# Attention turn of a fused attention and two-layer kernel: pooled work moved ahead of local work, sums moved to the end on DVE, and epsilon held in a column that a reduction adds

## The reference

```python
# attention: two parts, added
q_d, k_d, v_d = means over groups of 4 positions           # 144 positions
out_d = softmax(scale * q_d @ k_d.T) @ v_d                 # pooled part
out_up = repeat(out_d, 4)
scores = where(|i - j| < 4, scale * q @ k.T, -1e9)         # local part: a band of 7 keys
out_local = softmax(scores) @ v
x = out_up + out_local                                     # 2304 tokens x 512
# softmax everywhere: e = exp(s - max); e / (sum(e) + 1e-9)
# first layer: h = x @ w_in (512 x 2048); g = h * tanh(softplus(h)); y = g @ w_out
# second layer: h = y @ w_in (512 x 1024); h * softmax(h); layer norm * g_ln; @ w_out
```

## Time and profile before

| what | value |
|---|---|
| median of 3 runs | 707.73 us (707.36 to 709.15) |
| profiled execution, its own time | 707.11 us |
| its span in the trace | 705.3 us |
| PE busy | 678.3 us (96%), 5098 matmuls |
| DVE busy | 369.9 us (52%), 675 instructions |
| ACT busy | 262.5 us (37%) |
| POOL busy | 183.2 us (26%) |

### The profile page before, as it was taken

The page is one execution under the profiler, slowest core; times in us unless marked ns, Lnnn a source line. Parts: engine busy times, 40 slices in busy tenths (PEclk is TensorE's granted clock), DMA queues, the critical chain, the costliest instruction groups (busy, mean ns, idle before and its releaser), DMA issues.

```text
span 705.3 us, 12609 instructions
## 1 busy us (share of the span) xinstructions
PE 678.3 (96%) x5098; PEld 626.7 (89%) x5098; DVE 369.9 (52%) x675; ACT 262.5 (37%) x583; POOL 183.2 (26%) x220
## 2 busy tenths in 40 slices
PE   5878799999999999999999999999999999999998
PEld 5667689999999999999999999999778888888886
DVE  8999966642223222322232332664796667756671
ACT  5788874321112111211121112136564444535441
POOL 5989820000000000000000000574535434354100
PEclk9999999999999999999999999999999999999999
DMA  7887783000000000000000030002000000000001
GB/s 239 234 236 221 209 309 147 1 1 0 1 1 1 1 0 1 1 1 1 0 2 1 1 119 1 1 1 90 31 16 16 30 31 16 16 31 30 31 16 45
DMA packets 25657, 37.51 MB, mean 53 GB/s; under 512 B 2944, under 2 KB 13184, under 8 KB 25472
## 3 DMA queue, kind: packets, MB, share of 16 engines
q1 hardware_dynamic: 25600, 36.72, 16.3%
HBM read 31.99 MB, written 4.72 MB: 52 GB/s over the span
## 4 chain that ended last, share of the span: by engine, by line
PE 82%; DVE 10%; issue 3%; ACT 2%; POOL 2%; DMA 1%; SPq 0%; DVEq 0%; ACTq 0%; POOLq 0%
PE psum L685 28%; PE psum L671 28%; PE psum L778 12%; PE psum L755 11%; PE psum L764 2%; DVE prob L1110 2%; DVE mx L1107 1%; DVE xy L1134 1%; ACT pprob L839 1%; DVE den L1124 1%; DVE psum L1098 1%; POOL ylo L548 1%; DMA qkT<-kT_dram 1%; DVE so L1296 1%; DVE kd L1073 1%
## 5 line engine op out<-in xcount | busy, mean ns | idle before, releaser
L1193 DVE CAST ghi<-g_sb 128x384 fp32r<-128x384 f32 x96 | 39.6, 413 | 245.5 <-PE psum L685 188.8
L894 ACT ACTIVATE g_sb<-psum 128x384 f32<-128x384 f32 x96 | 47.0, 490 | 292.6 <-PE psum L671 288.3
L671 PE MATMUL psum<-xhi,whi 128*128 128x384 f32 x384 | 129.7, 338 | 1.3 <-ACT g_sb L894 0.7
L671 PE MATMUL psum<-xlo,whi 128*128 128x384 f32 x384 | 129.1, 336 | 0.0
L685 PE MATMUL psum<-ghi,whi 128*128 128x384 f32 x384 | 129.1, 336 | 0.0
L685 PE MATMUL psum<-ghi,wlo 128*128 128x384 f32 x384 | 129.1, 336 | 0.0
L671 PE MATMUL psum<-xhi,wlo 128*128 128x384 f32 x384 | 129.1, 336 | 0.0
L685 PE MATMUL psum<-glo,whi 128*128 128x384 f32 x384 | 129.1, 336 | 0.0
L520 POOL TENSOR_TENSOR t<-raw 128x1024 f32<-128x1024 f32 x1 | 2.6, 2609 | 350.3 <-PE psum L685 350.3
L671 PEld LDWEIGHTS psum<-xhi,whi 128*128 128x128 f32 x384 | 72.3, 188 | 2.4 <-ACT g_sb L894 1.2
L685 PEld LDWEIGHTS psum<-glo,whi 128*128 128x128 f32 x384 | 72.3, 188 | 0.1
(11 more groups left out here) (123 smaller groups left out, 1052.2 us busy)
## 6 DMA issues: line engine op xcount, KB each, us to landing
wraw<-w_dram SPq DMA_DIRECT2D x12, 512.0 KB, 8.1
qkT<-qT_dram SPq DMA_DIRECT2D x16, 288.0 KB, 3.7
qkT<-kT_dram SPq DMA_DIRECT2D x16, 288.0 KB, 5.1
out_dram<-ob SPq DMA_DIRECT2D x18, 256.0 KB, 2.0
v<-v_dram SPq DMA_DIRECT2D x16, 256.0 KB
vw<-v_dram SPq DMA_DIRECT2D x32, 128.0 KB, 3.2
wraw<-w_dram SPq DMA_DIRECT2D x16, 256.0 KB, 6.3
raw<-w_dram SPq DMA_DIRECT2D x1, 2048.0 KB, 7.2
```

What stands on the lines that cost most here:

```text
L671: ins = nc.tensor.matmul(bank, a[:, w], b[:, kdx, :], start=(kdx == 0 and n == 0), stop=(kdx == KD - 1 and n == 2))
L894: nc.scalar.activation(g_sb[:, f % HR, :], psum[:, HB1 + f % HB, 0:N1], ACT.Mish).then_inc(g_ok, 1)
L1193: nc.vector.tensor_copy(ghi[:, f % GR, :], g_sb[:, f % HR, :]).then_inc(ghi_ok, 1)
```

## The change

On POOL `den` is filled with epsilon first. It gets a last axis of two: column 0 takes the sums, column 1 keeps epsilon for the whole kernel. The addition becomes a reduction over that axis into a new tensor `dsum`, and the reciprocal reads `dsum`. ACT and DVE wait once for the fill. On PE the pooled scores go ahead of the local ones. On ACT `exp_pooled` goes ahead of the eviction of the older unit and of `exp_local`; what stood after `exp_pooled` in the queue now stands after `exp_local`. In turn 15 the rounding `split_x(0, KD - 1)` and `weights_in_high(1)` thus stand between `exp_pooled` and `exp_local`. On DVE `maxima_pooled` goes ahead of `subtract_local`, then the eviction of the older unit (in turn 15 only after the denominators, as before), `pool_keys`, `add_pooled` and `split_x`, and `sum_local` and `denominators` close the turn. `add_pooled(0, KD - 1)` of turn 14 and `weights_in_low` remain behind all of it.

```diff
--- before.py
+++ after.py
@@ -179,7 +179,8 @@
         identb = sb("identb", [P, P], BF16)
         mx = sb("mx", [P, 2, NP])
 
-        den = sb("den", [P, 2, NB + NPB])
+        den = sb("den", [P, 2, NB + NPB, 2])
+        dsum = sb("dsum", [P, 2, NB + NPB])
         rden = sb("rden", [P, 2, NB + NPB])
         pbias = sb("pbias", [P, NPB])
         one_end = top[0]
@@ -233,6 +234,7 @@
         zero_ok = sem("zero_ok")
         rest_ok = sem("rest_ok")
         ident_ok = sem("ident_ok")
+        eps_ok = sem("eps_ok")
         identb_ok = sem("identb_ok")
         band_ok = sem("band_ok")
         mask_ok = sem("mask_ok")
@@ -458,6 +460,7 @@
                 ins.then_inc(pool_own, 1)
                 pool.wait_ge(pool_own, n[0])
 
+            nc.gpsimd.memset(den[:], EPS_SM).then_inc(eps_ok, 1)
             own(nc.gpsimd.memset(ident[:], 0.0))
             nc.gpsimd.affine_select(out=ident[:], in_=ident[:], compare_op=ALU.not_equal, fill=1.0,
                                     base=0, pattern=[[-1, P]], channel_multiplier=1).then_inc(ident_ok, 1)
@@ -697,8 +700,8 @@
                     turn_pooled(u - LATE)
                     turn_local(u - LATE)
                 if u < UNITS:
+                    score_pooled(u)
                     score_local(u)
-                    score_pooled(u)
 
                 if u == UNITS:
                     pe.wait_ge(l_sub, UNITS)
@@ -829,6 +832,7 @@
         def _(act):
 
             nc.scalar.preload_act_table_set("natural_log_exp_and_others")
+            act.wait_ge(eps_ok, 1)
 
             def exp_pooled(u):
                 par = u % 2
@@ -838,7 +842,7 @@
                 for b in range(NPB):
                     ins = nc.scalar.activation(pprob[:, par, b, :], psum[:, SPB, b * POOLED:(b + 1) * POOLED], ACT.Exp,
                                                bias=pbias[:, b:b + 1], scale=SCALE / POOLF ** 2,
-                                               accum_out=den[:, par, NB + b:NB + b + 1])
+                                               accum_out=den[:, par, NB + b, 0:1])
                 ins.then_inc(p_exp, 1)
 
             def normalise_pooled(u):
@@ -899,6 +903,8 @@
                     copy_local(u - LATE)
                 if 0 < u <= UNITS:
                     normalise_pooled(u - 1)
+                if u < UNITS:
+                    exp_pooled(u)
                 if u == UNITS - 1:
                     split_x(0, KD - 1)
                     weights_in_high(1)
@@ -906,7 +912,6 @@
                     evict_pooled(u - LATE)
                 if u < UNITS:
                     exp_local(u)
-                    exp_pooled(u)
                 if u in ADDED:
                     split_x(0, ADDED.index(u))
                 if u == UNITS - 2:
@@ -1065,6 +1070,7 @@
             nc.vector.memset(v4[:, :, 1, :], 0.0).then_inc(rest_ok, 1)
 
             nc.vector.memset(psum[:, OB + 1, (NP - 1) * QB + QLAST:NP * QB], 0.0).then_inc(rest_ok, 1)
+            dve.wait_ge(eps_ok, 1)
             dve.wait_ge(ident_ok, 1)
             nc.vector.tensor_copy(identb[:], ident[:]).then_inc(identb_ok, 1)
 
@@ -1114,16 +1120,16 @@
             def sum_local(u):
                 par = u % 2
                 dve.wait_ge(l_exp, u + 1)
-                nc.vector.tensor_reduce(den[:, par, 0:NB], prob[:, par].rearrange("p i b k -> p (i b) k"),
+                nc.vector.tensor_reduce(den[:, par, 0:NB, 0], prob[:, par].rearrange("p i b k -> p (i b) k"),
                                         AX.X, ALU.add).then_inc(l_sum, 1)
 
             def denominators(u):
                 par = u % 2
                 dve.wait_ge(l_sum, u + 1)
                 dve.wait_ge(p_exp, u + 1)
-                nc.vector.tensor_scalar(den[:, par], den[:, par], EPS_SM, None, ALU.add).then_inc(den_ok, 1)
+                nc.vector.tensor_reduce(dsum[:, par], den[:, par], AX.X, ALU.add).then_inc(den_ok, 1)
                 dve.wait_ge(den_ok, u + 1)
-                nc.vector.reciprocal(rden[:, par], den[:, par]).then_inc(rden_ok, 1)
+                nc.vector.reciprocal(rden[:, par], dsum[:, par]).then_inc(rden_ok, 1)
 
             def evict_local(u):
 
@@ -1161,23 +1167,25 @@
 
             for u in range(UNITS + LATE):
                 if u < UNITS:
+                    maxima_pooled(u)
                     subtract_local(u)
-                    maxima_pooled(u)
-
-                    if u in ADDED:
-                        add_pooled(0, ADDED.index(u))
-                    if u - 1 in ADDED:
-                        split_x(0, ADDED.index(u - 1))
-                    if u == UNITS - 1:
-                        split_x(0, KD - 1)
-                    sum_local(u)
-                if u == UNITS - 1:
-                    denominators(u)
+
+
+                if LATE <= u != UNITS - 1:
+                    evict_local(u - LATE)
                 if u < UNITS - 1:
                     if u % 2 == 0:
                         pool_keys(u + 1)
+                if u in ADDED:
+                    add_pooled(0, ADDED.index(u))
+                if u - 1 in ADDED:
+                    split_x(0, ADDED.index(u - 1))
+                if u == UNITS - 1:
+                    split_x(0, KD - 1)
+                if u < UNITS:
+                    sum_local(u)
                     denominators(u)
-                if u >= LATE:
+                if u == UNITS - 1:
                     evict_local(u - LATE)
                 if u == UNITS - 2:
                     add_pooled(0, KD - 1)
```

## The result

The changed kernel takes 711.52 us (median of 11 runs, 710.0 to 714.0), the kernel before 708.35 us in the runs beside it (median of 11). The ratio is 1.0051, 95% interval 1.0037 to 1.0065: slower by 0.5%, which is 3.2 us by the medians and 3.6 by the ratio, and 0.1 us above the range. The profiled execution took 710.95 us with a span of 709.2, 3.9 us more than that of before.

What follows compares the result with a forecast made beforehand. DVE was taken as the bound, GpSimd 5% behind. Start +1.4, first scores +0.5, turns 4 to 11 -2.0, turns 12 and 13 -0.6, turn 15 +1.0: +0.3, so 707.4 us profiled, 708.0 median; range 703.8 to 711.4.

Steps and rivals of the forecast that it cites:

- What bounds the kernel: Attention stage up to 92.82 us: DVE is the bound, GpSimd 5% behind; a microsecond there moves the end by one.
- The epsilon: DVE's sixteen additions L1124 (mean 0.45 us) become reductions of 0.18, unstretched by GpSimd: 4.3 us less DVE time.
- The ring and four turns in 20.5: Steady turns: ACT's L848, L839, L874, L870 precede DVE's L1117 and reciprocal, releasing the next L848; four turns 20.5, not 21.5.
- The forecast's second reason: Odd turns: pooled scores wait for GpSimd's keys (L488), so the next turn starts at 4.55 us, not 4.45.
- The start: First units: PE waits for DVE's second pooling, so L1107(0) comes at 9.0; +1.4, plus 0.5 for slow first scores.
- rival C: The forecast's turns with PE slow also in the second unit: +0.9, 708.6 us; chance 0.12.
- Turn 14: `add_pooled(0,3)` and `weights_in_low(0)` keep their place behind the reciprocal and against GpSimd: change 0 from 6.95 us.
- Turn 15: ACT runs L870 last, so the reciprocal is done at 5.17 us into the turn instead of 4.16: +1.0.
- B: The ACT ring with GpSimd's lag leads: odd turns cost over 5.2, a cycle 21.5; +3.5, 711.2 us; chance 0.20.
- D: L1124's stall isn't removed but passes to L1154, L1149 and L1159: +2.1 on the forecast, 710.1 us; chance 0.08.
- A: DVE stays the bound and GpSimd's blocking falls away: a cycle takes 18.9 us; -4.1, 703.6 us; chance 0.22.

## Why the prediction was wrong, point by point

- **What bounds the kernel.** Right that the end follows DVE's `weights_in_low` (L1159) in the kernel before. Wrong that "the question is only when L1159 ends": after the change PE reached that group 1.0 us behind L1165 (95.91, group at 96.93).
- **The epsilon.** The reduction takes 0.179 to 0.182; 0.18 was taken. That it isn't stretched by GpSimd holds. Alone it shortens four turns by 1.6 us, more than the four additions of these turns lost (1.0): the stall didn't pass on to `split_x`, which got shorter too.
- **The ring and four turns in 20.5.** 20.67, the same in both cycles. Turns 4 to 13 gave 1.85 against the 2.6 forecast. What wasn't asked is whether the reduction without the new order would do better, and it does (19.92): the new order is a loss in itself. The ring through ACT isn't the reason in these turns. The forecast had DVE idle 0.3 us for L874 in each odd turn; from 27.9 to 80 us it never waited for it. It waited for the pooled scores (L590) five times, 1.1 us in all, and for L660 three times, 0.6 us, and the eviction took 0.76 instead of 0.70. The forecast's second reason, the pooled scores behind GpSimd's keys, is thus the one that the trace bears out, and it was sized too small: turns 5, 9 and 13 took 4.74 to 4.75 against 4.55. No run takes the orders of the single engines apart.
- **The start.** L1113 at 8.93 (forecast 9.0), the reciprocal done at 12.73 (12.79), and the second unit's L590 slow, as rival C had it; +2.15 against 1.4+0.5. The Trainium skill ("TensorE: Matmul & The Clock Gate", What's actually happening) has the array at half rate after idling; the durations here agree (1.23 us for 8 of L590, as in the first unit, against 0.71 in the third), the granted clock of 1.00 doesn't. As a term of the sum it was taken at full price, and that isn't shown: turn 0 in the old order moved L1104 of unit 1 by 2.4 us and the end by 0.35 to 1.5.
- **Turn 14: the step that failed first.** "Both in the same place behind the reciprocal and against GpSimd, 0" was the term; the turn measured +1.89. The moved eviction was costed at its 0.62, and nothing was said of the load in front of it. In the timeline of before L657 of unit 12 had already a wait of 0.69 for which the profile showed no releaser, and there the eviction stood last in the turn, where it held nobody. In the new order keys, sum and reciprocal stand behind it. The runs without v4 and with the weights later put the wait down to loads, the latter to the 512 KB of weights ahead of the windows of unit 12. What the moved eviction adds at the end by itself is read from the traces; the run that moved it back alone gave nothing in the median.
- **Turn 15: right in its own term, +0.94 against +1.0.** What failed is "nothing on PE hides it, since the group at 92.82 is what waits for it": another wait came later than that. The prediction followed L870 and L839 on ACT and costed L874 (L878 after) at 0.18, and missed that PE's `turn_pooled` waits for the eviction through `od_ok`. Measured: 1.5 to 2.5 us by moving it alone.
- **The rivals.** B forecast 711.2, near the 711.5, and by its mechanism it was wrong: from turn 4 to 13 no odd turn cost over 5.0, and a mean of four was 5.17. D is refuted for the steady turns: L1160's mean is 0.88 against 1.38 for the same work before. In turn 14 L1165 took 1.74 beside GpSimd's L508, where L1159 had taken 0.68, but `add_pooled` before it took 0.49 instead of 1.03. A needed cycles of 18.9.
- **In sum:** 707.4 was forecast for the profile and 710.95 came. At the group the forecast was +0.3 and +4.11 was measured: turn 14 (1.89), the join (0.98), the smaller gain of the turns (0.75) and the start (0.25), less 0.06 of turn 15, make the 3.81 between; 0.2 of it was regained behind the group.

Open stays why the windows land when they do. With turn 0 old PE stood at those of unit 11, issued from 68.01 on, which have no weights ahead of them; with the weights later those of unit 12, issued at 75.34, were used at 81.57. No run tells whether the bytes ahead of them or the issue slots count.

## What to carry to other kernels

An instruction that is moved forward in an in-order queue brings its own wait along: list every semaphore that it waits for, loads included, and who is queued behind it, and do the same for every semaphore that it releases. A stage that is steady for thirteen turns can be forecast to 0.2 us a cycle, and the result is still made in the two turns that differ, where weight loads, casts and the next stage come in. A wait of 0.7 us without a named releaser on an engine that isn't the bound is worth following, since it may become the bound once its consumer moves. And a wait taken away can come back as another one, on PE also as a lower clock: 1.1 and 1.7 us were saved before PE's transposes of turn 15, and 2.4 and 2.7 were paid behind them.

## What the runs showed of the hardware

- The granted clock of PE fell in the middle of the stage. In the run without v4 loads PE had been idle 3.4 us, then ran 6.5 us at a mean of 0.55, and 12 matmuls of 128x384 took 3.69 us instead of 2.09. With the weights later it was 3.36 us after 3.26 us without work, with the order alone 3.79 after 3.59, with turn 0 old 3.44 after 3.29; after an idle time of 2.07 us in the changed kernel they took 2.09. From L624 to the second group PE took 7.19 to 7.62 us in the first three and 6.36 in the fourth, against 4.78, so more was paid in clock than the wait saved. In the changed kernel the stretch from 85 to 90 us had 0.67, after waits of 1.40 (before the L624 at 77.82) and 1.77 us.
- At the start the view gives 1.00 for a stretch in which the same forms take 1.7 to 1.8 times as long as later (before: 1.31 against 0.75 us and 1.70 against 0.95), in the changed kernel until about 16.5 us (5 matmuls of L633 from 15.52 on in 1.24 against 0.71). The granted clock in the view did not show this.
- The length of the stand alone doesn't tell what the clock does: with turn 0 old it was 0.55 from 75 to 80 us after a stand of 1.98 us, while 2.07 us in turn 15 of the changed kernel left it at 1.00.
- The same TENSOR_TENSOR of 128x512 on DVE took 0.68 us in turn 14 of the kernel before, where GpSimd did nothing for most of it, and 1.74 us in turn 14 of the changed one, beside GpSimd's L508 and L500. The reduction of 26 elements kept within 179 to 182 ns in all 16.
